# Layernorm tiles transposed in squares by VectorE and through DRAM by DMA, with the w_out products one step later

## The chip, the cores and the metric

The kernel runs on one core of a Trainium2 chip. The metric is the device time of one execution in microseconds (us). The kernel before takes 496.76 us (median of three runs, 496.18 to 496.96). All views below come from one further, profiled execution of 496.89 us, whose traced span is 495.2 us.

## The reference

```python
# attention: batch 2, 8 heads, 768 positions, head_dim 64; keys 0..3 and a window of 128 are seen
scores = where(keep, q @ k.T / 8, -1e9);  a = softmax(scores);  x = a @ v    # -> 1536 tokens x 512
# first MLP: 512 -> 1024 -> 512
h = x @ w_in                      # 1536 x 1024
solu = h * softmax(h)
ln = (solu - mean) / sqrt(var + 1e-6) * g_ln
x2 = ln @ w_out                   # 1536 x 512
# second MLP: 512 -> 2048 -> 512
g = relu(x2 @ w2_in) ** 2
out = g @ w2_out                  # 1536 x 512
```

Everything is float32. Each product of the two MLPs is computed as three products in a rounded format: high by high, high by low and low by high, where "high" is the rounded operand and "low" is what the rounding left.

## The kernel before, in words

The 1536 tokens are 12 tiles of 128. Stage A (until about 224 us of the span) handles attention and the first MLP, in a pipeline written out by hand: `first_step`, `second_step`, then `step(t)` for t = 2 to 9 and `last_step` for t = 10. There is one such function for each engine, and each engine runs its list in order, waiting on semaphores. Stage B (`block_b`) is the second MLP, in three blocks of 512 tokens.

In `step(t)` three tiles are in work. With n = t + 1, TensorE does, in this order: the products of attention weights and values of tile n (`values`, `sink_values`); the transposes of tile t's layernorm (`transpose_ln`, 8 squares of 128 columns, from `u` in SBUF into PSUM); the first two of four pairs of score products of tile t + 2 (`score`); 7 of tile t's 24 w_out products (`project`, of 128x512 each); the other two pairs of scores; the 24 w_in products of tile n (`hidden`); 9 more w_out products; the transposes of tile t + 2's attention weights (`transpose_p`, `transpose_sinks`); the last 8 w_out products.

VectorE (`step`, line 950) does in one step: `square_x2(t - 1)`, which transposes the finished x2 tile in squares of 32x32; `normalize_hidden(t)`, two halves; `split_xT(n)`, the low part of tile n's attention output; three `split_lnT(t, part)`, the low parts of the transposed layernorm, read from PSUM; two `merge`s of scores and `row_max`; `split_q`; two more `merge`s and the second `row_max`; `normalize_p`, `hidden_max`, `split_k` and `gate_and_norm(n)`, which ends in the variance. ScalarE copies scores, rounds (`round_xT`, `round_lnT`), takes the exponentials and copies the transposed weights (`copy_pT`, `copy_sinksT`). GpSimd masks the transposed weights (`halves`) and takes the inverse deviation (`inverse_std`). Tiles 0 and 6 are "alone": they have no earlier keys, so that their score products are smaller and `halves` is left out. The transposed layernorms lie in PSUM banks that are otherwise those of x2 and h.

SyncE issues the loads of q, k and v and `move_x2(t)`: 16 DMAs from SBUF to SBUF, each of 16 KB in runs of 128 bytes, which put the 32x32 squares of x2 in their places in `x2T`, the operand of stage B.

Of the kernel before, what the change touches and what calls it, by code (L numbers as in the profile page):

```python
# [20 lines left out]
P = 128  # L21
# [15 lines left out]
EARLY = 2  # L37
WO_DVE = tuple(k for k in range(F1 // P) if k not in WO_POOL)
# [14 lines left out]
MOVES = 16 * QUADS * QUADS  # L53
# [3 lines left out]
LN_EPS, SM_EPS = 1e-6, 1e-9  # L57

# [11 lines left out]
def chunk_rows(h):  # L70

    return slice(h % 2 * D, (h % 2 + 1) * D), slice(h // 2 * P, (h // 2 + 1) * P)

# [61 lines left out]
def attention_moe_program(nc, qT, kT, v, w_in, w_out, g_ln, w2_in, w2_out, out):  # L135
# [6 lines left out]
    with ctx:  # L142
# [33 lines left out]

        def sbt(name, shape, dt=F32):
            return ctx.enter_context(nc.sbuf_tensor(name, shape, dt))
# [60 lines left out]
        never = sa("never", [P, N_SINK])  # L239
        first = flat(x2T)  # L240
# [50 lines left out]
        lnT_split, xT_split, x2T_moved = sem("lnT_split"), sem("xT_split"), [sem(f"x2T_moved{b}") for b in range(NB)]  # L291
# [4 lines left out]
        lnT_rounded, xT_rounded, x2_squared = sem("lnT_rounded"), sem("xT_rounded"), sem("x2_squared")  # L296
        x2T_rounded, x2T_split = sem("x2T_rounded"), sem("x2T_split")
# [7 lines left out]


# [16 lines left out]
        def _(sp):  # L323
# [19 lines left out]
            def move_x2(t):  # L343

                sp.wait_ge(x2_squared, t + 1)
                squares = squares_of(t).rearrange("p (c r b) -> p c r b", r=QUADS, b=SQ)
                for i in range(QUADS):
                    for r in range(QUADS):
                        sp.dma_start(x2T[r * SQ:(r + 1) * SQ, :, t * P + i * SQ:t * P + (i + 1) * SQ],  # L349
                                     squares[i * SQ:(i + 1) * SQ, :, r, :]).then_inc(x2T_moved[t // TB], 16)  # L350
# [33 lines left out]
            for n in range(3, NT):  # L384
                if n == 5:
                    load_q(n)
                if n >= 5:
                    move_x2(n - 5)
                if n != 5:
                    load_q(n)  # L390
                load_k(n)
                load_v(n - 1)
                if n == 4:
# [4 lines left out]
                if n in range(4, 4 + MC):  # L398
                    c = n - 4
                    sp.dma_start(w2in[:, c, :], w2_in[c * P:(c + 1) * P, :]).then_inc(w2in_loaded, 16)  # L400
            move_x2(NT - 5)
            load_v(NT - 1)
            move_x2(NT - 4)
            move_x2(NT - 3)
# [5 lines left out]
            move_x2(NT - 2)  # L410
            move_x2(NT - 1)
# [165 lines left out]
        def _(act):  # L577
# [54 lines left out]
            def round_lnT(t):  # L632
                done = len(LN_PARTS) * t
                for a, b, place, signals in ln_parts(t):
                    done += signals
                    act.wait_ge(lnT_done, done)
                    nc.scalar.activation(lnT_hi[:, a:b, :], place.rearrange("p (k q) -> p k q", q=P),
                                         ACT.Copy).then_inc(lnT_rounded, signals)
# [17 lines left out]
            def step(t, nxt=True):  # L656
# [7 lines left out]
                if nxt:  # L664
                    copy_earlier(t + 2, 0)
                    copy_earlier(t + 2, 1)
                    bias(t + 2, 0)
                    softmax_exp(t + 2, 0)
                    copy_earlier(t + 2, 2)
                    softmax_exp(t + 2, 1)  # L670
                    copy_earlier(t + 2, 3)
                    softmax_exp(t + 2, 2)
                    softmax_exp(t + 2, 3)
                    finish(t)
# [14 lines left out]
            def first_step():  # L689

                round_xT(1)
                copy_earlier(2, 0)
                copy_earlier(2, 1)
                round_w_out(1, 5)
                copy_earlier(2, 2)
                copy_earlier(2, 3)
                bias(2, 0)
                for h in range(HG):
                    softmax_exp(2, h)
                round_lnT(0)  # L700
                round_w_out(5, len(WO_DVE))
                bias(2, 1)
                for h in range(HG, H):
                    softmax_exp(2, h)
                round_k(3)
                copy_pT(2, 0)
                copy_pT(2, 1)
                hidden_exp(1)
                copy_sinksT(2)

            def second_step():

# [11 lines left out]
                round_lnT(1)  # L724
                finish(1)
# [42 lines left out]
            def round_x2T(blk):  # L768
                cols = slice(blk * BLK, (blk + 1) * BLK)
                act.wait_ge(x2T_moved[blk], TB * MOVES)  # L770
                nc.scalar.activation(x2T_hi[:, :, cols], x2T[:, :, cols], ACT.Copy).then_inc(x2T_rounded, 1)
# [6 lines left out]
            step(NT - 2, nxt=False)  # L778
# [18 lines left out]
            round_lnT(NT - 1)  # L797
# [20 lines left out]
        def _(dve):  # L818
# [99 lines left out]
            def split_lnT(t, part):  # L918
                done = len(LN_PARTS) * t + sum(signals for _, _, _, signals in ln_parts(t)[:part + 1])
                a, b, place, signals = ln_parts(t)[part]  # L920
                dve.wait_ge(lnT_rounded, done)
                nc.vector.tensor_tensor(lnT_lo[:, a:b, :], place.rearrange("p (k q) -> p k q", q=P),  # L922
                                        lnT_hi[:, a:b, :].bitcast(F32), ALU.subtract).then_inc(lnT_split, signals)
# [6 lines left out]
            def square_x2(t):  # L930

                dve.wait_ge(x2_done, t + 1)
                if 0 < t < NT - 1:
                    dve.wait_ge(x2T_moved[(t - 1) // TB], (t - 1) % TB * MOVES + MOVES)
                nc.vector.transpose(squares_of(t), x2_ps[:, :]).then_inc(x2_squared, 1)
# [148 lines left out]
            square_x2(NT - 3)  # L1084
            normalize_hidden(NT - 2)
            split_xT(NT - 1)
            for part in range(len(ln_parts(NT - 2))):
                split_lnT(NT - 2, part)
# [47 lines left out]
        def _(pe):  # L1136
            mm = nc.tensor.matmul

            def score(n, p):
# [6 lines left out]
                if merges(n) and p == 0:  # L1146
                    pe.wait_ge(merged, merges(n))
                if p == 0 and sink_tiles(n):
# [97 lines left out]
            def transpose_ln(t):  # L1246
                if t:
# [9 lines left out]
            def project(t, first, last):  # L1257
                for k, i in x2_products[first:last]:
# [30 lines left out]
            def step(t):  # L1289


                n = t + 1
                values(n, 0)
# [3 lines left out]
                if alone(n):  # L1297
                    score(t + 2, 0)
                    score(t + 2, 1)
                transpose_ln(t)  # L1300
                if not alone(n):
                    score(t + 2, 0)
                    score(t + 2, 1)
# [10 lines left out]
                project(t, 16, 24)  # L1314

            def last_step():
# [4 lines left out]
                sink_values(n)  # L1321
                transpose_ln(n - 1)
                hidden(n, 0, 24)
# [27 lines left out]
            def second_step():  # L1351
# [17 lines left out]
                project(1, 0, 16)  # L1369
# [3 lines left out]
                project(1, 16, 24)  # L1373
# [125 lines left out]
```

## Time and profile before

| what | us |
|---|---|
| median of three runs | 496.76 |
| profiled execution | 496.89 |
| its span | 495.2 |
| TensorE busy | 483.3 (98%) |
| VectorE busy | 284.5 (57%) |
| ScalarE busy | 200.9 (41%) |
| GpSimd busy | 94.3 (19%) |
| stage A, about | 0 to 224 |

Busy time is averaged over the whole span. Stage B is nearly all TensorE, so that VectorE's 57% says little of stage A, where the profile's forty slices show it at eight or nine tenths busy. TensorE's granted clock is at full speed in every slice. The profile's chain that ended last is 82% TensorE and 10% VectorE.

### The profile page before, as it was taken

What the parts mean: (1) busy time and instruction counts of PE and PEld (TensorE: products, weight loads), DVE (VectorE), ACT (ScalarE), POOL (GpSimd) and SP (SyncE); (2) the same over time, 40 slices, a digit from 0 to 9 for tenths busy, and PEclk for the clock granted to TensorE, in tenths of its full rate; (3) what the DMA queues carried; (4) which work ended last, traced back from release to release, by engine and by line L of the source; (5) the groups of instructions that cost most, each with busy time, mean ns of one, the idle gap of its engine ahead of it and who ended that gap; (6) DMA issues with size and microseconds to landing.
All of it is one profiled execution on the core that took longest, in us unless ns stands there. A gap on an engine that the chain in (4) does not pass through costs nothing.

```text
span 495.2 us, 7334 instructions
## 1 busy us (share of the span) xinstructions
PE 483.3 (98%) x2644; PEld 392.8 (79%) x2644; DVE 284.5 (57%) x512; ACT 200.9 (41%) x531; POOL 94.3 (19%) x138
## 2 busy tenths in 40 slices
PE   7989989999999999999999999999999999999997
PEld 5667767888778888878888888888888888888885
DVE  3999888898898888775673554323222332222232
ACT  3667646545655663532334253322112221211221
POOL 2555042120022112267970000000000000000000
PEclk9999999999999999999999999999999999999999
DMA  8921343352222221119100000010000001000002
GB/s 222 309 79 43 134 106 104 124 161 64 59 60 76 53 48 34 17 30 344 29 3 0 1 0 1 34 51 0 0 0 0 0 23 63 0 1 0 0 1 85
DMA packets 39717, 29.21 MB, mean 59 GB/s; under 512 B 29256, under 2 KB 29256, under 8 KB 39176
## 3 DMA queue, kind: packets, MB, share of 16 engines
q1 hardware_dynamic: 39224, 28.30, 19.7%
q10 hardware_dynamic: 464, 0.53, 0.5%
q8 instruction: 18, 0.29, 0.2%
q14 instruction: 11, 0.09, 0.1%
HBM read 22.52 MB, written 3.15 MB: 52 GB/s over the span
## 4 chain that ended last, share of the span: by engine, by line
PE 82%; DVE 10%; SPq 2%; ACT 2%; DMA 1%; issue 1%; POOL 0%; DVEq 0%
PE score_ps L1424 26%; PE h_ps L1438 13%; PE w_ps L1262 10%; PE h_ps L1224 9%; PE wt_ps L1438 7%; PE w_ps L1438 7%; PE o_ps L1194 3%; SPq L349 2%; PE score_ps L1166 2%; PE wt_ps L1174 2%; DVE nmax L850 1%; DVE wo_lo L946 1%; PE wt_ps L1166 1%; PE h_ps L1252 1%; DMA x2T<-kT 1%; DVE prob L915 1%
## 5 line engine op out<-in xcount | busy, mean ns | idle before, releaser
L1424 PE MATMUL score_ps<-x2T_hi,w2in_hi 128*128 (+1 forms) x192 | 74.8, 389 | 0.0
L1424 PE MATMUL score_ps<-x2T_hi,w2in_lo 128*128 (+1 forms) x192 | 74.7, 389 | 0.0
L1424 PE MATMUL score_ps<-x2T_lo,w2in_hi 128*128 (+1 forms) x192 | 74.7, 389 | 0.0
L1099 DVE TENSOR_TENSOR e<-e 128x512 f32<-128x512 f32 x24 | 17.1, 712 | 82.1 <-ACT e L785 82.1
L1099 DVE TENSOR_TENSOR sq<-relu 128x512 f32<-128x512 f32 x24 | 17.7, 738 | 77.9 <-ACT relu L785 77.9
L785 ACT ACTIVATE relu<-score_ps 128x512 f32<-128x512 f32 x24 | 14.4, 598 | 94.2 <-PE score_ps L1424 94.2
L785 ACT ACTIVATE e<-score_ps 128x512 f32<-128x512 f32 x24 | 14.4, 600 | 92.5 <-PE score_ps L1424 92.5
L1424 PEld LDWEIGHTS score_ps<-x2T_hi,w2in_hi 128*128 128x128 f32 x192 | 36.1, 188 | 7.5
L1424 PEld LDWEIGHTS score_ps<-x2T_lo,w2in_hi 128*128 128x128 f32 x192 | 36.0, 188 | 7.5
L1424 PEld LDWEIGHTS score_ps<-x2T_hi,w2in_lo 128*128 128x128 f32 x192 | 36.0, 188 | 7.4
L610 ACT ACTIVATE prob<-sm,nbias 128x132 f32<-128x132 f32 (+1 forms) x96 | 37.9, 396 | 0.5
L1224 PE MATMUL h_ps<-w_hi,xT_hi 128*128 128x512 f32 x88 | 35.6, 405 | 1.3 <-DVE xT_lo L927 1.3
L1262 PE MATMUL w_ps<-wo_hi,lnT_hi 128*128 128x512 f32 x88 | 35.4, 402 | 0.5 <-DVE lnT_lo L922 0.5
L1262 PE MATMUL w_ps<-wo_lo,lnT_hi 128*128 128x512 f32 x88 | 35.2, 400 | 0.0
L1224 PE MATMUL h_ps<-w_hi,xT_lo 128*128 128x512 f32 x88 | 34.4, 391 | 0.0
L1224 PE MATMUL h_ps<-w_lo,xT_hi 128*128 128x512 f32 x88 | 34.4, 391 | 0.0
L1262 PE MATMUL w_ps<-wo_hi,lnT_lo 128*128 128x512 f32 x88 | 34.4, 391 | 0.0
L629 ACT ACTIVATE e<-h_ps,nhmax 128x512 f32<-128x512 f32 x24 | 16.3, 685 | 24.8 <-DVE nhmax L860 24.8
L572 POOL TENSOR_TENSOR w2in_lo<-w2in,w2in_hi 128x512 fp32r<-128x512 f32 x16 | 23.3, 1454 | 1.3
L1224 PEld LDWEIGHTS h_ps<-w_hi,xT_hi 128*128 128x128 f32 x88 | 16.5, 187 | 6.1 <-issue 1.1
L1262 PEld LDWEIGHTS w_ps<-wo_hi,lnT_hi 128*128 128x128 f32 x88 | 16.5, 188 | 5.4 <-DVE lnT_lo L922 1.3
L452 POOL CAST p_sink<-prob 128x64 fp32r<-128x64 f32 x10 | 2.4, 239 | 90.2 <-DVE prob L915 83.3
(182 smaller groups left out, 1105.7 us busy)
## 6 DMA issues: line engine op xcount, KB each, us to landing
w2in<-w_in SPq DMA_DIRECT2D x4, 1024.0 KB, 5.5
w2out<-w_out SPq DMA_DIRECT2D x8, 512.0 KB, 7.5
V<-v SPq DMA_DIRECT2D x12, 256.0 KB, 2.7
x2T<-x SPq DMA_DIRECT2D x176, 16.0 KB, 1.9
k_raw<-kT SPq DMA_DIRECT2D x20, 132.0 KB, 2.8
q_raw<-qT SPq DMA_DIRECT2D x20, 128.0 KB, 2.8
w2in<-w_in SPq DMA_DIRECT2D x4, 512.0 KB, 7.9
w2in<-w_out SPq DMA_DIRECT2D x2, 1024.0 KB, 13.3
```

Of the source, the lines that this page charges most:

```text
L349: sp.dma_start(x2T[r * SQ:(r + 1) * SQ, :, t * P + i * SQ:t * P + (i + 1) * SQ], squares[i * SQ:(i + 1) * SQ, :, r, :]).then_inc(x2T_moved ...
L572: nc.gpsimd.tensor_tensor(w2in_lo[:, :, fs], w2in[:, :, fs], w2in_hi[:, :, fs].bitcast(F32), ALU.subtract).then_inc(w2in_split, 1)
L610: nc.scalar.activation(prob[:, h, seen(n)], sm[:, h, seen(n)], ACT.Exp, bias=nbias[:, h:h + 1], scale=SCALE, accum_out=psum_row[:, h:h + 1 ...
L629: nc.scalar.activation(e[:, cols], h_ps[:, cols], ACT.Exp, bias=nhmax[:, :], scale=1.0, accum_out=hsum[:, half:half + 1]).then_inc(h_exped, 1)
L785: nc.scalar.activation(relu[f % 2], h2_ps[f % 2], ACT.Relu).then_inc(relu_ready, 1)
L1099: nc.vector.tensor_tensor(sq[f % 2], relu[f % 2], relu[f % 2], ALU.mult).then_inc(sq_ready, 1)
L1166: done = mm(score_banks(n, p)[:, j, cols], qs[rows], ks[rows], start=(n < 2 or i == 0), stop=(n < 2 or i == len(products) - 1))
L1194: last = mm(o_ps[rows, cols], V[:, slot, h * D:(h + 1) * D], pT[:, g, j * P:(j + 1) * P], start=(g == 0 and part == 0 and i < 2), stop=(al ...
L1224: done = mm(h_ps[:, cols], xs[:, c, :], ws[:, c, cols], start=(c == 0 and k == 0), stop=(c == MC - 1 and k == 2))
L1262: done = mm(x2_ps[:, :], ls[:, k, :], ws[:, k, :], start=(k == 0 and i == 0), stop=(k == C1 - 1 and i == 2))
L1424: done = mm(h2_ps[f % 2], ws[:, c, fs], xs[:, c, bass.ts(blk, BLK)], start=(c == 0 and i == 0), stop=(c == MC - 1 and i == 2))
L1438: done = mm(y_ps[q], gs[f % 2][:, qs], ws[:, f, :], start=(f == 0 and i == 0), stop=(f == C2 - 1 and i == 2))
```

## The change

For tiles 2 to 9 (`carried`) TensorE no longer transposes the layernorm. Instead VectorE transposes `u` in 32x32 squares into a new SBUF tile `uT` (`square_u`, two instructions of 128x512, after `split_xT`); SyncE stores it to DRAM in two DMAs (`store_u`) and loads it back in four DMAs in runs of 512 bytes, so that the squares fall in their places in `lnT_raw` (`load_lnT`). ScalarE rounds and VectorE splits from `lnT_raw`, in SBUF, one step later. The w_out products of tile t - 1 stand in `step(t)`: 3 before `hidden`, 15 after it, 6 after the transposes. The second step does 12 of tile 1's 24 (`LEAD`), step 2 the other 12, and the last step does tile 9's 24 and tile 10's 24. `score(t + 2, 0)` and `(1)` now open TensorE's step, ahead of `values`. Tiles 0, 1, 10 and 11 are transposed by TensorE as before.

x2 also goes through DRAM: 4 DMAs a tile (`store_x2`) write runs of 128 bytes, and 4 DMAs a block of four tiles load them (`load_x2T`), where there were 16 DMAs a tile.

```diff
-MOVES = 16 * QUADS * QUADS
+MOVES = 16 * QUADS
+def carried(t):
+    return EARLY <= t < NT - 2
@@ SyncE
-            def move_x2(t):
+            def store_x2(t):
                 sp.wait_ge(x2_squared, t + 1)
                 for i in range(QUADS):
-                    for r in range(QUADS):
-                        sp.dma_start(x2T[...], squares[...]).then_inc(x2T_moved[t // TB], 16)
+                    sp.dma_start(x2_dram[:, :, :, cols]..., squares_of(t)[i * SQ:(i + 1) * SQ, :]...
+                                 ).then_inc(x2_stored, 16)
+            def store_u(t):
+                for half in range(2):
+                    sp.wait_ge(u_squared, 2 * (t - EARLY) + half + 1)
+                    sp.dma_start(u_dram[t, half * QUADS:(half + 1) * QUADS, :, :, :]..., uT[:, half, :]
+                                 ).then_inc(u_stored, 16)
+            def load_lnT(t):
+                sp.wait_ge(u_stored, 32 * (t - EARLY + 1))
+                sp.wait_ge(lnT_split, len(LN_PARTS) * t)
+                for r in range(QUADS):
+                    sp.dma_start(lnT_raw[r * SQ:(r + 1) * SQ, :, :], u_dram[t, :, :, r, :]...).then_inc(lnT_loaded, 16)
+            for t in range(EARLY, NT - 2):
+                if t > EARLY:
+                    store_x2(t - 2)
+                load_v(t + 2)
+                store_u(t)
+                if t + 4 < NT:
+                    load_q(t + 4)
+                load_lnT(t)
+                if t + 4 < NT:
+                    load_k(t + 4)
@@ ScalarE, step(t)
+                if t > EARLY:
+                    round_lnT(t - 1, 0)
+                copy_earlier(t + 2, 0)
+                copy_earlier(t + 2, 1)
                 if t + 3 < NT:
                     round_q(t + 3)
                 round_xT(n)
-                round_lnT(t)
...
+                    round_lnT(t - 1, 1)
+                    round_lnT(t - 1, 2)
@@ VectorE
+            def square_u(t):
+                if t > EARLY:
+                    dve.wait_ge(u_stored, 32 * (t - EARLY))
+                for half in range(2):
+                    dve.wait_ge(ln_ready, 2 * t + half + 1)
+                    nc.vector.transpose(uT[:, half, :], u[:, cols].rearrange("p (k r b) -> p r k b", r=QUADS, b=SQ)
+                                        ).then_inc(u_squared, 1)
@@ VectorE, step(t)
-                square_x2(t - 1)
+                if t > EARLY:
+                    square_x2(t - 2)
+                    split_lnT(t - 1, 0)
+                merge(t + 2, 0)
+                merge(t + 2, 1)
                 normalize_hidden(t)
                 split_xT(n)
-                for part in range(len(LN_PARTS)):
-                    split_lnT(t, part)
-                merge(t + 2, 0)
-                merge(t + 2, 1)
+                square_u(t)
+                if t > EARLY:
+                    split_lnT(t - 1, 1)
+                    split_lnT(t - 1, 2)
                 row_max(t + 2, 0)
@@ TensorE, step(t)
+                first = LEAD if t == EARLY else 0
+                score(t + 2, 0)
+                score(t + 2, 1)
                 values(n, 0)
                 values(n, 1)
...
-                transpose_ln(t)
-                project(t, 0, 7)
                 score(t + 2, 2)
                 score(t + 2, 3)
-                pe.wait_ge(lnT_split, len(LN_PARTS) * (t + 1))
+                project(t - 1, first, first + 3)
+                pe.wait_ge(u_ready, 2 * t + 2)
                 hidden(n, 0, 24)
-                project(t, 7, 16)
+                project(t - 1, first + 3, 18)
                 transpose_p(t + 2, 0)
                 transpose_p(t + 2, 1)
...
-                project(t, 16, 24)
+                project(t - 1, 18, 24)
@@ TensorE, last_step
                 sink_values(n)
+                project(n - 2, 0, 24)
                 transpose_ln(n - 1)
@@ TensorE, second_step
-                project(1, 0, 16)
+                project(1, 0, LEAD)
                 transpose_p(3, 0)
                 transpose_p(3, 1)
                 transpose_sinks(3)
-                project(1, 16, 24)
```

## Rows read from the trace of the kernel before

**Rows 1.** Busy time by stretch: stretch, length, then PE, PEld, DVE, ACT, POOL, clock.

```profile
157.27:174.87 17.60, 17.60 (x129) 14.39 (x127) 14.90 (x33) 10.23 (x35) 3.56 (x7) 1.00 0.24 62
```

**Rows 2.** The chain that ended last, step 3: start, length, what, instructions.

```profile
89.06 0.25 PE w_ps L1252 x2
89.30 0.66 PE h_ps L1252 x6
89.96 0.56 PE score_ps L1166 x5
90.52 0.36 PE wt_ps L1166 x6
```

**Rows 3.** VectorE's timeline, step 8: start, length, instruction, idle before and its releaser.

```profile
177.62 0.41 DVE L922 TENSOR_TENSOR lnT_lo<-w_ps,lnT_hi 128x256 fp32r<-128x256 f32 x1
177.95 1.01 DVE L922 TENSOR_TENSOR lnT_lo<-h_ps,lnT_hi 128x256 fp32r<-128x256 f32 x2
178.88 0.44 DVE L838 COPY_PREDICATED sm<-own_seen,score_ps 128x256 f32<-128x256 uint32 x1
...
182.60 0.70 DVE L850 TENSOR_REDUCE nmax<-sm 128x4 f32<-128x528 f32 x1
...
185.67 0.17 DVE L910 TENSOR_SCALAR z_eps<-psum_row 128x4 f32<-128x4 f32 x1 [0.73 <-ACT prob L610]
...
192.31 0.70 DVE L935 STREAM_TRANSPOSE x<-w_ps 128x512 f32<-128x512 f32 x1
```

**Rows 4.** VectorE's timeline in the second step and at the start of step 2.

```profile
53.49 1.00 DVE L894 TENSOR_SCALAR u<-u,moments,rstd 128x512 f32<-128x512 f32 x2
54.41 0.43 DVE L838 COPY_PREDICATED sm<-own_seen,score_ps 128x256 f32<-128x256 uint32 x1
...
55.21 0.70 DVE L850 TENSOR_REDUCE nmax<-sm 128x4 f32<-128x528 f32 x1
55.83 0.68 DVE L904 TENSOR_TENSOR QL<-q_raw,QH 128x512 fp32r<-128x512 f32 x1
56.43 0.71 DVE L935 STREAM_TRANSPOSE x<-w_ps 128x512 f32<-128x512 f32 x1
...
70.03 0.72 DVE L935 STREAM_TRANSPOSE x<-w_ps 128x512 f32<-128x512 f32 x1 [0.50 <-DMA x2T<-x]
70.67 0.96 DVE L894 TENSOR_SCALAR u<-u,moments,rstd 128x512 f32<-128x512 f32 x2
```

**Rows 5.** ScalarE's timeline around the start of step 2.

```profile
66.77 0.29 ACT L622 ACTIVATE p_sinkT<-score_ps 96x128 fp32r<-96x128 f32 x1
...
70.47 0.60 ACT L645 ACTIVATE xT_hi<-o_ps 128x512 fp32r<-128x512 f32 x1 [2.89 <-PE o_ps L1211]
```

**Rows 6.** TensorE's timeline, end of the second step and start of step 2.

```profile
63.85 1.04 PE L1174 MATMUL wt_ps<-ident,prob 128*128 128x128 f32 x8
...
67.28 0.66 PE L1194 MATMUL o_ps<-pT_own,V 128*64 128x128 f32 x8 [0.44 <-POOL pT_own L462]
```

**Rows 7.** VectorE's timeline: second row maximum of step 2, x2 squares of steps 3, 10.

```profile
77.39 0.70 DVE L850 TENSOR_REDUCE nmax<-sm 128x4 f32<-128x528 f32 x1
...
87.44 0.70 DVE L935 STREAM_TRANSPOSE x<-w_ps 128x512 f32<-128x512 f32 x1
...
209.89 0.70 DVE L935 STREAM_TRANSPOSE x<-w_ps 128x512 f32<-128x512 f32 x1
```

**Rows 8.** The chain that ended last, last step.

```profile
213.02 5.69 PE h_ps L1224 x24
218.71 5.44 PE w_ps L1262 x24
```

**Rows 9.** The page's DMA queues: kind, packets, MB, share of 16 engines.

```profile
q1 hardware_dynamic: 39224, 28.30, 19.7%
```

**Rows 10.** The page's DMA issues: count, KB each, median us to landing.

```profile
V<-v SPq DMA_DIRECT2D x12, 256.0 KB, 2.7
```

**Rows 11.** SyncE's queue: start, time of the issues, count.

```profile
158.56 11.16 SPq L349 DMA_DIRECT2D x2T<-x  x16
```

More of the change, by code:

```diff
@@ L72, in chunk_rows, with transposed_before @@
     return slice(h % 2 * D, (h % 2 + 1) * D), slice(h // 2 * P, (h // 2 + 1) * P)
+def transposed_before(t):
+    return sum(not carried(i) for i in range(t))
 def flat(x):
@@ L304, in attention_moe_program, with lnT_chunks, in_squares @@
         block = ctx.enter_context(nc.Block())
+        def lnT_chunks(t, part):
+            a, b, place, _ = ln_parts(t)[part]
+            if not carried(t):
+                return place.rearrange("p (k i b) -> p k i b", i=QUADS, b=SQ)
+            half, k = a // (C1 // 2), a % (C1 // 2)
+            return lnT_raw[:, half * QUADS:(half + 1) * QUADS, k * SQ:(k + b - a) * SQ].rearrange("p i (k b) -> p k i b", b=SQ)
+        def in_squares(x):
+            return x.rearrange("p k (i b) -> p k i b", b=SQ)
         def squares_of(t):
@@ L383, in _, with load_w2_in @@
             load_v_sink(1)
[L384 to L393, printed above, removed]
+            def load_w2_in(c):
+                if c == 0:
                     sp.wait_ge(w_split, MC - 1)
@@ L397, in _ @@
                     sp.wait_ge(wo_split_pool, len(WO_POOL))
[L398 to L404, printed above, removed]
+                sp.dma_start(w2in[:, c, :], w2_in[c * P:(c + 1) * P, :]).then_inc(w2in_loaded, 16)
+            for n in range(3, 5):
+                load_q(n)
+                load_k(n)
+                load_v(n - 1)
+            load_w2_in(0)
+            load_q(5)
+            store_x2(0)
+            load_k(5)
+            for t in range(EARLY, NT - 2):
[8 more added lines that the diff above has]
+                    load_k(t + 4)
+                if t - EARLY + 1 < MC:
+                    load_w2_in(t - EARLY + 1)
+                if t == TB + 2:
+                    load_x2T(0)
+            store_x2(NT - 4)
+            store_x2(NT - 3)
+            load_x2T(1)
             sp.wait_ge(h_done, 2 * NT)
@@ L662, in step @@
                 round_xT(n)
-                round_lnT(t)
[L664 to L674, printed above, removed]
+                if t > EARLY:
+                    round_lnT(t - 1, 1)
+                    round_lnT(t - 1, 2)
+                copy_earlier(t + 2, 2)
+                copy_earlier(t + 2, 3)
+                bias(t + 2, 0)
+                for h in range(HG):
+                    softmax_exp(t + 2, h)
+                finish(t)
             def finish(t):
@@ L699, in first_step @@
                     softmax_exp(2, h)
-                round_lnT(0)
+                for part in range(2):
+                    round_lnT(0, part)
                 round_w_out(5, len(WO_DVE))
@@ L723, in second_step @@
                 softmax_exp(3, 3)
-                round_lnT(1)
+                for part in range(2):
+                    round_lnT(1, part)
                 finish(1)
@@ L775, in round_w2out @@
                 nc.scalar.activation(w2out_hi[:, f, :], w2out[:, f, :], ACT.Copy).then_inc(w2out_rounded, 1)
-            step(NT - 2, nxt=False)
+            round_lnT(NT - 3, 0)
+            round_xT(NT - 1)
+            round_lnT(NT - 3, 1)
+            round_lnT(NT - 3, 2)
+            act.wait_ge(x2_done, NT - 2)
+            for part in range(len(ln_parts(NT - 2))):
+                round_lnT(NT - 2, part)
+            act.wait_ge(lnT_split, len(LN_PARTS) * (NT - 2))
             act.wait_ge(o_done, sink_tiles(NT))
@@ L796, in _ @@
             chain(0, 0)
-            round_lnT(NT - 1)
+            for part in range(len(LN_PARTS)):
+                round_lnT(NT - 1, part)
             act.wait_ge(wo_half_read, 1)
@@ L1246, in transpose_ln @@
             def transpose_ln(t):
-                if t:
+                if t and t != NT - 2:
                     pe.wait_ge(x2_squared, t)
@@ L1257, in project @@
             def project(t, first, last):
+                if t > EARLY - 1 and first == 0:
+                    pe.wait_ge(x2_squared, t)
                 for k, i in x2_products[first:last]:
```

76 lines of the change are left out of this document (50 added, 26 removed).

## The prediction

> **What bounds the kernel now.** I read the busy time by stretch first, then the chain of waits, then each engine's own timeline. In an ordinary step of stage A TensorE is busy for 17.60 of 17.60 us, VectorE for 14.90, at a granted clock of 1.00 [rows 1]. So TensorE sets the step, and the eight layernorm transposes stand on its chain: 0.25 + 0.66 = 0.91 us [rows 2], about 1.0 with the gaps beside them. But VectorE's 14.90 is not 2.70 of free time. Between its work lie waits for ScalarE, such as 0.73 us ahead of z_eps [rows 3], which stay whatever TensorE does, because ScalarE in turn waits for VectorE's row maxima. The question is what VectorE's own loop takes once TensorE needs less.
>
> **TensorE's new step.** It loses 1.0 us and nothing is added: some 16.5 us, if it never waits.
>
> **VectorE's new step.** I lay its list out in the new order, by distances from start to start.
> - From the second row maximum to the x2 squares of the next step nothing changes in order: 182.60 to 192.31, 9.71 us, waits for ScalarE included [rows 3].
> - Squares of x2: 70.03 to 70.67, 0.64 [rows 4].
> - Split of layernorm part 0: 177.62 to 177.95, 0.33 [rows 3]. It now reads SBUF, not PSUM; the split of q, from SBUF, takes 0.60 for twice the width [rows 4], so I change nothing.
> - First two merges: a pair takes 0.80 with the wait of the maximum behind it [rows 4]; no maximum follows here, so twice 0.33, 0.66.
> - Both halves of the normalization: 53.49 to 54.41, 0.92 [rows 4]. The wait for the inverse deviation is covered by the splits and merges now ahead of it.
> - Split of the attention output, as wide as the split of q: 0.60.
> - New: two squares of u. No row shows a transpose that reads SBUF with gaps. The nearest row is the same instruction from PSUM, 0.64, and I take it, twice 1.28. Below, half the normalization of the same tile, 0.46; above, 0.92, twice that, were the gaps to halve the speed. Ends for eight steps of two: 2.9 us less, 4.5 us more.
> - Splits of parts 1 and 2: 177.95 to 178.88, 0.93 [rows 3].
> - First row maximum 0.62, split of q 0.60 [rows 4].
> - Last two merges, with the wait: 0.80. The waits for the score copies that stood here before go, since the scores are made much earlier.
>
> Sum ahead of the second maximum: 0.64 + 0.33 + 0.66 + 0.92 + 0.60 + 1.28 + 0.93 + 0.62 + 0.60 + 0.80 = 7.38. With 9.71 that is 17.09 us, more than TensorE's 16.5. VectorE becomes the bound, and an ordinary step goes from 17.60 to 17.1: 0.5 us gained, not 1.0. TensorE will stand about 0.6 us at the top of each step, for the copy of the transposed sinks, which ScalarE makes behind the exponentials of h, which wait for VectorE.
>
> **Steps 2 to 9.** At the end of the second step TensorE loses 12 products, but gains no time by it: its next scores need the copy that ends at 67.06 [rows 5], so step 2 opens at 67.2 in place of 67.28 [rows 6]. Score pairs take 0.56 + 0.36 = 0.92 [rows 2], and the values and sinks some 3.2 before (67.28 to 70.47, with waits for GpSimd that shrink by the 0.9 us of later start). The rounded attention output is there at about 71.2, its split starts at 71.3. From there 0.60 + 1.28 + 0.62 + 0.60 + 0.80 (step 2 has no squares of x2 and no layernorm splits) gives the second maximum at 75.2, where it was at 77.39, and the x2 squares of step 3 at 75.2 + 9.71 = 84.9, where they were at 87.44 [rows 7]: 2.5 us ahead. Of the seven steps that follow, five are ordinary, 0.5 each; the one that scores the alone tile was already loose on VectorE, I give it 0.2, and the one behind it 0.4. That is 3.1, and the squares of step 10 come at 209.89 - 5.6 = 204.3.
>
> **The last step gives it back.** TensorE has 24 products more there: 5.44 us [rows 8]. Before, it did from 209.89 to 218.71 + 5.44 = 224.15. Now: squares, part 0, normalization, attention split, part 1, that is 0.64 + 0.33 + 0.92 + 0.60 + 0.33 = 2.82, and 0.5 for the wait on the attention output and the way to TensorE, releases its third chunk at 207.6. Then 18 products (0.227 each, 4.09), the transposes (0.91), the w_in products (5.69) and 24 products (5.44): 223.8. Stage A ends 0.3 us earlier. Of some 8 us of transposes taken away, TensorE spends most as waiting: about 5 where products were moved out of the second step and step 2, which VectorE bounds, the rest at 0.6 a step.
>
> **DMA.** SyncE issues 16 pieces of x2 in 11.16 us [rows 11], 0.70 each. In their place come 4 + 2 + 4, 7 us: its queue gets freer. Counted from the x2 squares: u is squared at 4.7, its store issued by 5.5 and landed by 8.2 (2.7 for 256 KB [rows 10]). In the queue q's two loads stand between; they wait for the split of q (6.9) and end at 8.3. The four layernorm loads are issued by 11.1 and landed by 13.8; ScalarE wants them at 17.1. Slack 3.3 us, so I cost the trip at nothing. V, ahead of u in the queue, waits for values made 3 us into the step: no delay. The k loads and w2_in behind it have a step of room. Stage B's x2 blocks are stored a step or more before they are read.
>
> **Small pieces into DRAM.** A tile's x2 is 2048 runs of 128 bytes, 128 for each of 16 DMA engines. All packets of the queue take 19.7% of 16 x 495.2 us over 39224 packets, 0.040 us on average [rows 9]: 5.1 us a tile, with u's store behind them. That alone moves u's landing from 8.2 to 11.3 and the layernorm's to 16.8: just in time. Above, 2048 pieces were issued in 11.16 us without piling up, so at most 0.087 each. The Trainium skill, "DMA: Bandwidth & Descriptors", section "Why small descriptors are slow (HBM only)", says that small descriptors cost extra where DRAM is an end, and not between SBUF and SBUF; its "Specifications" say that below 512 bytes the engine reads, modifies and writes. No row before has such a write; the rule points to the rival below, and its own time would be that rival's.
>
> **Rivals.**
> - *TensorE stays the bound (faster).* If the u squares are nearer 0.46, or VectorE's order absorbs more, the step is 16.5 and seven steps gain 0.6 more: 4.2, so 492.4. For it: VectorE's 14.90 busy plus 1.28 is 16.2. Against it: the sum of 17.09.
> - *The layernorm comes late (slower).* It decides above 0.044 us for a 128-byte write. ScalarE's round and VectorE's split of part 0 stand ahead of the merges in both queues, so every us of delay is one of the step. At 0.052 it is 1 us in seven steps: 503.6. Against it: short pieces are surely below the average of a queue whose other packets carry 2 KB.
> - *The clock falls.* TensorE finishes the second step's products 0.9 us before 63.85, so that after transposes of 1.0 it stands from about 64.0 to 67.2, 3.2 us; its pauses before were under 1 us here, at clock 1.00. At 1.2 GHz the scores and values that follow take some 3 us more, and I give it 3 us: 499.6. The Trainium skill, "TensorE: Matmul & The Clock Gate", section "Why this matters for your kernels", warns of idle gaps between bursts of matmuls. By that rule this pause is what speaks against the change.
> - *VectorE and GpSimd hinder each other more* than in these rows: the shift puts the splits beside GpSimd's masks and, in the last step, its w2_in casts. 0.3 us a step and 1 at the end: 499.6.
>
> **How the numbers follow.** 496.89 - 0.3 = 496.6 for an execution like the profiled one; that one lies 0.13 above the median, so 496.5. Chances: forecast 0.40 (own range 495.0 to 498.5, as 0.1 us of a square moves it by 1.6), TensorE bound 0.32, late layernorm 0.13, clock 0.07, hindrance 0.08. Changes under 0.2% (1.0 us) can't be told from none here. The first splits into 0.08 faster, 0.28 same, 0.04 slower; with 0.31 of the second that makes faster 0.39; same 0.29; slower 0.32. The range goes from 492.4 to 501.0, the upper end of the squares' cost, which leaves out most of the late case and a tail below.
>
> **What the profile after would show.** The forecast: ordinary steps of 17.1 us; VectorE without waits but ScalarE's 0.7; TensorE waiting 0.6 at each step's first score and 3 us before step 2; stage A ending near 223.8; u squares of 0.64 to 0.70. It is wrong if steps are 16.5, if ScalarE waits for DMA before rounding part 0, if the clock shows under 1.00 near 67 us, or if the last step is shorter than 19 us from its x2 squares.

## The result and the profile after

The changed kernel takes 499.54 us (median of five runs, 498.81 to 500.19) against 496.81 us for the kernel before (five runs, 496.18 to 496.96): ratio 1.0057, 95% interval 1.0042 to 1.0072. It is slower by 2.7 us, where I had forecast no difference. Its profiled execution took 500.16 us, span 498.1 us, granted clock 0.997 over the span.

Both profiled executions have GpSimd's inverse deviation of tile 1 at 50.36 us, so their times can be set side by side from there. To compare kernels whose executions start differently, I use one length throughout, "stage A from tile 1": from the start of that instruction to the first product of the second MLP, as the chain that ended last gives it (227.00 after, 224.15 before). It is 173.79 us before and 176.64 after, 2.85 more. Another 0.4 lies outside the span (2.06 us in place of 1.69).

The busy time by stretch (stretch, length, then PE, PEld, DVE, ACT, POOL, each with its instructions, the granted clock, DMA share, GB/s):

```profile
64.00:67.20 3.20, 0.18 (x2) 0.00 (x0) 2.90 (x6) 2.57 (x7) 0.64 (x1) 1.00 0.18 47
67.20:69.00 1.80, 1.72 (x24) 1.62 (x26) 1.69 (x4) 1.05 (x3) 1.70 (x3) 0.90 0.19 67
69.00:72.00 3.00, 3.00 (x27) 2.67 (x23) 2.11 (x7) 0.21 (x1) 1.41 (x3) 0.50 0.00 0
155.22:172.46 17.24, 16.86 (x123) 13.63 (x121) 15.87 (x35) 10.39 (x35) 3.55 (x8) 1.00 0.66 159
```

The last row answers to [rows 1]: the ordinary step shrank from 17.60 to 17.24 us, TensorE is no longer busy all the time, and VectorE is busy for 15.87. The other rows are the surprise. TensorE pauses ahead of step 2. In the pause its granted clock still reads 1.00 (2.4 GHz); in the first 1.8 us of work behind it the mean is 0.90, and then it is 0.50, the 1.2 GHz level, for three microseconds. TensorE's timeline there (start, length, instruction, idle before and its releaser), to be set against [rows 6]:

```profile
63.91 0.27 PE L1302 MATMUL score_ps<-ident,p_sink 128*96 128x128 f32 x1
67.28 0.39 PE L1266 MATMUL score_ps<-KH,QH 64*128 64x260 f32 x2 [3.10 <-ACT p_sinkT L687]
...
68.19 0.74 PE L1294 MATMUL o_ps<-pT_own,V 128*64 128x128 f32 x8
68.72 1.07 PE L1294 MATMUL o_ps<-pT_earlier,V 128*64 128x128 f32 x8
```

A group of eight value products takes 1.07 us in place of 0.66 [rows 6], and VectorE stands for 1.83 us until their rounded result is there (its timeline at step 2 and at the x2 squares of step 3; the rows answer to [rows 7]):

```profile
73.04 0.69 DVE L1017 TENSOR_TENSOR xT_lo<-o_ps,xT_hi 128x512 fp32r<-128x512 f32 x1 [1.83 <-ACT xT_hi L713]
73.65 1.30 DVE L1012 STREAM_TRANSPOSE uT<-u 128x512 f32<-128x512 f32 x2
...
76.86 0.70 DVE L929 TENSOR_REDUCE nmax<-sm 128x4 f32<-128x528 f32 x1
...
79.92 0.17 DVE L989 TENSOR_SCALAR z_eps<-psum_row 128x4 f32<-128x4 f32 x1 [0.69 <-ACT prob L675]
...
86.84 0.72 DVE L1025 STREAM_TRANSPOSE x<-w_ps 128x512 f32<-128x512 f32 x1
```

The two squares of u, the one instruction whose cost no row of before showed, take 1.30 from first start to last end: 73.65 to the maximum at 74.87 is 1.22, 0.61 each.

The other loss is in the last step. VectorE's timeline there, then GpSimd's:

```profile
206.18 0.72 DVE L1025 STREAM_TRANSPOSE x<-w_ps 128x512 f32<-128x512 f32 x1
206.82 0.38 DVE L1001 TENSOR_TENSOR lnT_lo<-lnT_raw,lnT_hi 128x256 fp32r<-128x256 f32 x1
207.12 2.41 DVE L973 TENSOR_SCALAR u<-u,moments,rstd 128x512 f32<-128x512 f32 x2
209.46 0.68 DVE L1017 TENSOR_TENSOR xT_lo<-o_ps,xT_hi 128x512 fp32r<-128x512 f32 x1
210.06 2.11 DVE L1001 TENSOR_TENSOR lnT_lo<-lnT_raw,lnT_hi 128x256 fp32r<-128x256 f32 x2
```

```profile
207.21 0.61 POOL L635 CAST w2in_hi<-w2in 128x512 fp32r<-128x512 f32 x1 [0.35 <-PE o_ps L1311]
207.90 1.34 POOL L637 TENSOR_TENSOR w2in_lo<-w2in,w2in_hi 128x512 fp32r<-128x512 f32 x1
209.20 0.80 POOL L635 CAST w2in_hi<-w2in 128x512 fp32r<-128x512 f32 x1
210.08 1.53 POOL L637 TENSOR_TENSOR w2in_lo<-w2in,w2in_hi 128x512 fp32r<-128x512 f32 x1
```

The same normalization takes 1.00 for its two halves in the last step before and 0.99 in an ordinary step after; here it takes 2.41 beside GpSimd's work on w2_in, and the two splits 2.11 in place of 0.98. The split in between, 0.68, is not touched; it has one operand in PSUM. The Trainium skill, "SBUF — State Buffer", section "SBUF: two separate sides", says that VectorE and GpSimd exclude each other on a shared pair of ports when VectorE runs in a mode of two ports, or reads two operands from SBUF while GpSimd reads SBUF too. These rows agree with it: the two groups that grew have all their operands in SBUF, the one that didn't grow has not. e2 tests it. What it cost is on the chain that ended last, which answers to [rows 8] (start, length, what):

```profile
207.20 2.33 DVE u L973 x2
...
210.52 1.66 PE w_ps L1364 x6
...
212.22 3.02 PE w_ps L1364 x12
215.24 0.87 PE score_ps L1352 x8
216.11 5.46 PE h_ps L1324 x24
221.56 5.44 PE w_ps L1364 x24
227.00 4.09 PE score_ps L1523 x18
```

The page's DMA issues (count, KB each, median us to landing) answer to [rows 10]:

```profile
u_dram<-uT SPq DMA_DIRECT2D x16, 256.0 KB, 3.3
lnT_raw<-u_dram SPq DMA_DIRECT2D x32, 128.0 KB, 2.7
...
x_dram<-x SPq DMA_DIRECT2D x44, 64.0 KB, 2.2
```

A 64 KB piece that is written in runs of 128 bytes lands in 2.2 us, and in steps 3 to 9 neither TensorE, VectorE nor ScalarE waits for a DMA.

### The profile page after: what moved, and what is told of

The parts are those of the page before. It is cut to its first block, busy times and chain, and to the rows that moved or that the text cites. A ratio compares the mean times of both kernels' runs of the same rounds, so it can differ in the third digit from the quotient of the medians.

```text
span 498.1 us, 7178 instructions
## 1 busy us (share of the span) xinstructions
PE 479.3 (96%) x2580; PEld 388.7 (78%) x2580; DVE 293.6 (59%) x528; ACT 201.6 (40%) x531; POOL 93.1 (19%) x138
## 4 chain that ended last, share of the span: by engine, by line
PE 62%; DVE 28%; ACT 6%; issue 3%; POOL 1%; DVEq 0%; POOLq 0%; ACTq 0%
PE score_ps L1523 26%; PE h_ps L1537 13%; PE wt_ps L1537 7%; PE w_ps L1537 7%; ACT prob L675 4%; PE w_ps L1364 3%; DVE nmax L929 3%; DVE bstat L951 2%; DVE u L944 2%; DVE sm L917 2%; DVE lnT_lo L1001 2%; PE h_ps L1324 2%; DVE prob L994 2%; DVE uT L1012 2%; DVE hmax L934 1%
## 5 line engine op out<-in xcount | busy, mean ns | idle before, releaser
L1197 DVE TENSOR_TENSOR e<-e 128x512 f32<-128x512 f32 x24 | 17.1, 712 | 82.1 <-ACT e L863 82.1
L1364 PE MATMUL w_ps<-wo_hi,lnT_hi 128*128 128x512 f32 x88 | 36.4, 414 | 2.0 <-DVE lnT_lo L1001 1.9
L1324 PEld LDWEIGHTS h_ps<-w_hi,xT_hi 128*128 128x128 f32 x88 | 16.5, 188 | 7.9 <-issue 4.7
L1364 PEld LDWEIGHTS w_ps<-wo_hi,lnT_lo 128*128 128x128 f32 x88 | 16.5, 188 | 3.6
```

What stands on the lines that cost most here:

```text
L1197: nc.vector.tensor_tensor(sq[f % 2], relu[f % 2], relu[f % 2], ALU.mult).then_inc(sq_ready, 1)
L1324: done = mm(h_ps[:, cols], xs[:, c, :], ws[:, c, cols], start=(c == 0 and k == 0), stop=(c == MC - 1 and k == 2))
L1364: done = mm(x2_ps[:, :], ls[:, k, :], ws[:, k, :], start=(k == 0 and i == 0), stop=(k == C1 - 1 and i == 2))
```

## The experiments

My theory after the comparison: the step's gain is real, and the loss has two places, the clock behind the pause before step 2 and the meeting of VectorE and GpSimd in the last step. The rival was that the pause and the meeting are only symptoms, and that VectorE's added work delays everything. Later runs ask what bounds the shorter step. All kernels but the two marked "from the kernel before" start from the changed kernel.

| kernel | stage A from tile 1, us | ordinary step, us | median, us | ratio to before, interval |
|---|---|---|---|---|
| before | 173.79 | 17.60 | 496.81 | |
| after | 176.64 | 17.24 | 499.54 | 1.0057 (1.0042 to 1.0072) |
| e1 idle products | 175.13 | 17.25 | 499.79 | 1.0053 (1.0029 to 1.0078) |
| e2 GpSimd later | 174.76 | 17.24 | 498.22 | 1.0019 (1.0005 to 1.0033) |
| e3 both | 173.63 | 17.24 | 497.83 | 1.0020 (1.0004 to 1.0037) |
| e4 one square of u | 171.04 | 16.66 | 494.26 | 0.9942 (0.9918 to 0.9966) |
| e5 from before, q on GpSimd | 173.87 | 17.58 | 496.51 | 0.9990 (0.9977 to 1.0003) |
| e7 e2 + 18 products in the second step | 173.68 | 17.24 | 497.17 | 1.0007 (0.9990 to 1.0023) |
| e8 e7 + q on GpSimd | 171.58 | 17.01 | 496.18 | 0.9984 (0.9960 to 1.0008) |
| e9 from before, x2 by DRAM | 173.42 | 17.57 | 496.34 | 0.9990 (0.9975 to 1.0005) |
| e10 e7 + late splits | 168.65 | 16.46 | 492.33 | 0.9919 (0.9891 to 0.9948) |
| e12 e8 + early maximum | 171.78 | 16.89 | 494.25 | 0.9949 (0.9930 to 0.9968) |
| e11 e7 + all three | 168.18 | 16.47 | 490.86 | 0.9882 (0.9848 to 0.9917) |

The first two columns are of one profiled execution each; each ratio is to the runs of the kernel before on the same chip.

**e1: idle products fill the pause.** Thirteen products of 128x512 whose results nobody reads, behind the second step's transposes.

```diff
                 transpose_sinks(3)
+                for _ in range(13):
+                    mm(o_ps[:, :], wo_hi[:, 0, 0:P], wo_hi[:, 1, :], start=True, stop=True)
```

> The changed kernel, with 13 idle products of 128x512 put into TensorE's pause at the end of the second step; they write o_ps, which the values of the next tile start afresh. Theory (the pause of 3.1 us lets the clock fall to 0.50 for about 4 us, and that makes the attention output of step 2 late): the clock stays at 1.00 from 67 to 73 us, the values of step 2 take about 2.0 us in place of 3.2, the second row maximum of step 2 comes at 75.3 in place of 76.9, and the whole takes 1.6 us less than the changed kernel's 499.5, so 497.9. Rival (the values were late for GpSimd's masks, the clock is a side matter): the maximum stays near 76.9 and the time at 499.5.

The clock stays up, and the value products have their old length:

```profile
67.00:71.00 4.00, 4.00 (x60) 3.57 (x58) 3.63 (x10) 2.00 (x5) 2.34 (x5) 1.00 0.15 38
```

```profile
63.43 3.22 PE L1474 MATMUL o_ps<-wo_hi 128*128 128x512 f32 x13
66.76 0.39 PE L1266 MATMUL score_ps<-KH,QH 64*128 64x260 f32 x2
...
68.16 0.61 PE L1294 MATMUL o_ps<-pT_earlier,V 128*64 128x128 f32 x8
```

Counted from tile 1, the split of the attention output starts 1.66 us sooner (70.90 - 49.88 = 21.02, against 73.04 - 50.36 = 22.68). Of that, 0.5 is lost at once: the split of q behind it takes 1.16 us in place of 0.68, since it now falls beside GpSimd's work on the values of the sinks (VectorE's line, then GpSimd's):

```profile
73.30 1.16 DVE L983 TENSOR_TENSOR QL<-q_raw,QH 128x512 fp32r<-128x512 f32 x1
```

```profile
72.62 1.30 POOL L570 TENSOR_TENSOR v_sink<-v_sink_raw,v_sink 32x512 fp32r<-32x512 f32 x1
```

So the second row maximum of step 2 comes 1.2 us sooner, and that much of stage A is the clock's. Stage A is 1.5 us shorter; the other 0.3 falls in step 3, where hz and hz_eps (told below) are shorter. The total does not show the gain and misses the 497.9 that I expected: of the 499.79 us, 2.67 lie outside the span (median), against 1.99 in the changed kernel, and the median span is 496.9 against 497.6.

**e2: GpSimd's w2_in work later.** It now waits for the last step's splits.

```diff
             pool.wait_ge(w2in_loaded, 16 * MC)
+            pool.wait_ge(lnT_split, len(LN_PARTS) * (NT - 2))
```

> The changed kernel, with GpSimd's split of w2_in beginning only when VectorE has split the layernorm of tile 9. Theory (in the last step the two halves of the normalization take 2.3 us in place of 0.9, and the two splits 2.1 in place of 0.9, because GpSimd's casts and subtractions hold SBUF against them): they take 0.9 each again, stage A ends 1.7 us earlier, 497.8. Rival (the last step hangs on TensorE's 24 more products anyway, and a later w2_in makes stage B late): no gain, 499.5 or more.

Stage A is 1.9 us shorter, and the total 1.3. VectorE's timeline, then the chain:

```profile
205.70 0.72 DVE L1026 STREAM_TRANSPOSE x<-w_ps 128x512 f32<-128x512 f32 x1
206.34 0.38 DVE L1002 TENSOR_TENSOR lnT_lo<-lnT_raw,lnT_hi 128x256 fp32r<-128x256 f32 x1
206.64 0.99 DVE L974 TENSOR_SCALAR u<-u,moments,rstd 128x512 f32<-128x512 f32 x2
207.55 0.68 DVE L1018 TENSOR_TENSOR xT_lo<-o_ps,xT_hi 128x512 fp32r<-128x512 f32 x1
208.15 1.01 DVE L1002 TENSOR_TENSOR lnT_lo<-lnT_raw,lnT_hi 128x256 fp32r<-128x256 f32 x2
```

```profile
208.62 4.37 PE w_ps L1365 x18
```

The squares of x2 to the release of the products are 2.92 us (205.70 to 208.62), where the changed kernel has 4.34 and I had forecast 3.3; and the 18 products run in 4.37 in place of 4.72 with a wait inside. The length of the instructions came back by moving GpSimd alone, so the meeting is the cause. The total, 498.2, is 0.4 above the 497.8 that I expected.

**e3: both edits.**

> Both edits of the two runs before. Theory: the two costs lie at different ends of stage A and add up, 499.5 - 3.3 = 496.2, the forecast's 496.5 within 0.5 us. Rival (they overlap, or something else is late next): above 497.5.

In stage A the two costs add: 176.64 - 173.63 = 3.01 us, e2's 1.88 and 1.13 more for the clock. The median spans say the same: 496.35 in e2, 495.2 here. That leaves the stage 0.16 us shorter than before; the forecast was 0.3. The total still stands 0.20% above before, since 2.53 us lie outside the span, against 1.74 for the kernel before; the median spans, 495.2 and 495.3, are equal. The 497.83 lies above the 496.2 that I expected, and on the rival's side of 497.5. The spans show that nothing in stage A was late next; what the rival did not name is the time outside the span.

**e4: only one of the two squares of u** in steps 2 to 9. It leaves out the upper half of these layernorms; SyncE's store, not shown, sends the lower half twice.

```diff
-                for half in range(2):
-                    dve.wait_ge(ln_ready, 2 * t + half + 1)
-                    nc.vector.transpose(uT[:, half, :], ...).then_inc(u_squared, 1)
+                dve.wait_ge(ln_ready, 2 * t + 2)
+                nc.vector.transpose(uT[:, 0, :], ...).then_inc(u_squared, 2)
```

> The changed kernel with one square transpose of u a step in place of two; it leaves out the upper half of the layernorm of tiles 2 to 9 and stores the lower half twice. Theory (VectorE's own list is the bound of every step): each of the eight steps falls by the 0.61 us of the instruction, ordinary ones from 17.24 to 16.63, and the whole to 494.6. Rival (TensorE, or ScalarE's exponentials, set the step): less than 0.15 us a step, above 498.3.

A step of 16.66 in place of 17.24: 0.58 less for an instruction that stands 0.61 in VectorE's order. So VectorE sets the changed step, and TensorE, busy for 16.60 of 16.60 here, is the next bound right behind it:

```profile
155.00:171.60 16.60, 16.60 (x119) 13.54 (x118) 15.23 (x34) 10.40 (x35) 3.55 (x7) 1.00 0.48 129
```

**e5: the kernel before, with seven splits of q on GpSimd.** It takes 0.60 us a step from VectorE. The other half of the edit, not shown, has GpSimd make the split behind the inverse deviation.

```diff
                 row_max(t + 2, 0)
-                if t + 3 < NT:
-                    split_q(t + 3)
```

> The kernel before, with the split of q of seven steps (0.60 us each) taken from VectorE and given to GpSimd behind the normalization. Theory (in the kernel before TensorE alone sets the step): no gain, steps stay at 17.60 and the whole within 0.5 us of 497.0. Rival (VectorE is a bound there too): 0.3 us or more a step, 495 or less.

Nothing moves: steps of 17.58, TensorE busy for all of them. In the kernel before TensorE alone set the step.

```profile
157.00:174.60 17.60, 17.60 (x127) 14.42 (x126) 14.29 (x32) 10.15 (x36) 4.86 (x9) 1.00 0.24 57
```

**e7: half the pause, without idle work.** On top of e2 (its line is not shown), six more w_out products of tile 1 come into the second step, behind its transposes, and step 2 keeps only its last six (the guard that skips the others there is not shown).

```diff
-LEAD = 12
+LEAD = 18
                 project(1, 0, 12)
                 transpose_p(3, 0)
                 transpose_p(3, 1)
                 transpose_sinks(3)
+                project(1, 12, LEAD)
```

> The changed kernel with the later w2_in of GpSimd, and TensorE's pause filled with useful work: 6 of tile 1's w_out products stand behind the transposes of the second step, the last 6 at the end of step 2. Theory (the pause lets the clock fall, whatever fills it keeps it): clock 1.00 from 67 to 73 us, second row maximum of step 2 as in the kernel with idle products, stage A as long as in the kernel before within 0.5 us, and no product more than before, so 497.1. Rival (a pause of 1.7 us is enough for the clock to fall, or the products delay the scores): 498.2, as without the filling.

TensorE's pause is 1.7 us, its clock stays at 1.00, and the value products behind it take 0.60 to 0.66 us:

```profile
66.26 0.39 PE L1267 MATMUL score_ps<-KH,QH 64*128 64x260 f32 x2 [1.69 <-ACT p_sinkT L688]
```

Here too the split of q takes 1.14 us beside GpSimd. Stage A is as long as in e3, and 1.92 us lie outside the span, not 2.53: 497.17, the same as before. With both losses mended the change is worth nothing, as the forecast had it.

**e8: e7 with the seven splits of q on GpSimd.**

> The kernel of the run before this one, with the split of q of seven steps given to GpSimd. Theory (here VectorE sets the step): each of the seven loses 0.60 us, 17.24 to 16.64, and the whole comes to 497.1 - 4.2 = 492.9, faster than both kernels. Rival (TensorE's own list, 16.5 by the forecast, or GpSimd's hold on SBUF takes it back): 495 or more.

A miss. The step lost 0.23 us, not the 0.60 that left VectorE's list. VectorE's timeline says why:

```profile
158.35 0.70 DVE L936 TENSOR_REDUCE nmax<-sm 128x4 f32<-128x528 f32 x1
159.60 0.17 DVE L996 TENSOR_SCALAR z_eps<-psum_row 128x4 f32<-128x4 f32 x1 [0.55 <-ACT prob L682]
...
161.78 0.17 DVE L996 TENSOR_SCALAR z_eps<-psum_row 128x4 f32<-128x4 f32 x1 [0.45 <-ACT prob L682]
```

A wait of 0.55 for ScalarE's exponentials is new, ahead of the first z_eps; the one ahead of the second fell from 0.69 to 0.45. Together 0.31 us of the 0.60 became waiting; a last 0.06 I did not trace. The exponentials start only at the first row maximum, and nothing ahead of that had become shorter. The rival that GpSimd's hold on SBUF takes the gain back is out: beside GpSimd's split of q (1.29 us) the two squares of u keep their 1.29. VectorE's list is no sum: it is a loop through ScalarE.

**e9: the kernel before, with only x2 through DRAM.** The move of x2 (`store_x2`, `load_x2T`) alone, in place of 16 DMAs a tile.

> The kernel before with x2 alone going through DRAM, as in the change: 4 stores a tile in runs of 128 bytes and 4 loads a block; the layernorms are transposed by TensorE. Theory (x2's way is hidden whichever it takes): no change, within 0.5 us of 497.0, steps of 17.60. Rival (short writes to DRAM hold up q, k and v behind them): slower by 1 us or more, ScalarE waiting for q.

Steps of 17.57 and a ratio of 0.999: that part of the change costs nothing and brings nothing.

**e10: e7 with the layernorm's second and third splits later.** They leave the place ahead of the row maxima, where they take 0.91 us, for the one behind the first `normalize_p`, where VectorE waits for ScalarE's exponentials.

```diff
                 square_u(t)
-                if t > EARLY:
-                    split_lnT(t - 1, 1)
-                    split_lnT(t - 1, 2)
...
                 normalize_p(t + 2, 0)
+                if t > EARLY:
+                    split_lnT(t - 1, 1)
+                    split_lnT(t - 1, 2)
```

> The kernel with the filled pause and the later w2_in, with VectorE's splits of layernorm parts 1 and 2 (0.93 us) moved from ahead of the first row maximum to behind the first half's normalized weights. Theory (a step is the loop of VectorE from row maximum to ScalarE's exponentials and back; what stands ahead of the maxima counts in full, what stands behind them fills the wait of 0.69): the wait ahead of the second z_eps goes, an ordinary step falls by 0.69 from 17.24 to 16.55, seven steps give 4.8, so 492.3. Rival (VectorE's load is the bound as a sum, wherever it stands): no change, 497.1. Second rival (TensorE's w_out products now wait for the splits): 497.5 or more.

As forecast: the step is 16.46 us and the total 492.33. TensorE is busy for all of a step here (16.46 of 16.46 us), so that its own list is the bound again, at the 16.5 of the forecast; what VectorE's loop alone would now take can't be read from this run. The splits stand where the wait was, and the second z_eps waits for nothing:

```profile
157.00 0.17 DVE L990 TENSOR_SCALAR z_eps<-psum_row 128x4 f32<-128x4 f32 x1
...
158.05 1.02 DVE L1002 TENSOR_TENSOR lnT_lo<-lnT_raw,lnT_hi 128x256 fp32r<-128x256 f32 x2
...
159.59 0.16 DVE L990 TENSOR_SCALAR z_eps<-psum_row 128x4 f32<-128x4 f32 x1
```

**e12: e8 with the first row maximum directly behind the first two merges.** If the exponentials' late start is what e8 ran into, this should free it.

```diff
                 merge(t + 2, 1)
+                row_max(t + 2, 0)
                 normalize_hidden(t)
...
-                row_max(t + 2, 0)
                 merge(t + 2, 2)
```

> The kernel with the split of q on GpSimd (steps of 17.01), with the first row maximum moved from behind the layernorm splits to directly behind the first two merges. Theory of the loop: the wait for the exponentials that replaced the split of q (0.55 ahead of the first z_eps) goes, since they now begin 4 us earlier; the split's 0.60 then counts in full and a step falls from 17.01 to 16.64, seven steps 2.6 us, so 493.6. Rival (VectorE's list as a sum): no change, 496.2.

The wait ahead of the first z_eps is gone, but 0.73 us now stand ahead of the second, and the step is 16.89, 0.12 less than in e8, where I had expected 0.37 less (16.64). A miss as well: taking one wait away brought the next one out. The total, 494.25, is 1.9 lower than e8's, while stage A is no shorter in the profiled executions (171.78 against 171.58). Executions of one kernel differ by that much (493.96 to 499.94 in e8), so I take only the step from it.

**e11: e7 with all three edits**, the splits of q on GpSimd, the early maximum and the late splits.

> All edits together: filled pause, later w2_in, split of q on GpSimd, first row maximum behind the merges, layernorm splits behind the normalized weights. Theory: VectorE's loop would need 17.24 - 0.69 - 0.60 = 15.95, so TensorE is the bound again at the 16.5 of the forecast; 497.1 - 7 x 0.74 = 491.9, faster than both kernels by 5 us. Rival (ScalarE's chain or the copy of the sinks sets another bound near 17.0): 495.5 or more.

```profile
155.00:172.00 17.00, 17.00 (x121) 14.12 (x120) 15.65 (x35) 10.95 (x38) 4.98 (x8) 1.00 0.49 133
```

490.86 us (490.62 to 491.53), 1.2% below the kernel before and the best version here. TensorE is busy all the time again, at 16.47 us a step, with VectorE at 15.65 of 17.00. The step is no shorter than e10's, and can't be, since TensorE bounds both: the late splits alone reach that bound, and what the other two edits would give on top is not shown.

## Why the prediction was wrong

**TensorE bounds the kernel before: right.** e5 takes 0.60 us a step from VectorE and the step stays.

**An ordinary step of 17.1, set by VectorE: right.** It measured 17.24, and e4 shows whose bound it is. From the squares of x2 to the second row maximum it takes 7.25 (155.08 to 162.33) where my sum has 7.38; the squares of u were 1.22 for two against 1.28. The stretch from the second row maximum to the next squares of x2 was 9.99, not 9.71 [rows 3]. That row was one of the shortest: in the kernel before the stretch already runs from 9.68 to 10.06 in steps 3 to 9, and I took the row of step 8 for all. VectorE and GpSimd meet in this stretch as well, as VectorE's and then GpSimd's timeline of an ordinary step after show:

```profile
170.08 0.62 DVE L946 SCALAR_TENSOR_TENSOR hz<-hsum 128x1 f32<-128x1 f32 x1
...
171.40 0.58 DVE L956 SCALAR_TENSOR_TENSOR hz_eps<-hz 128x1 f32<-128x1 f32 x1
```

```profile
170.05 0.64 POOL L531 TENSOR_SCALAR_AFFINE_SELECT pT_earlier<-pT_earlier 128x512 f32<-128x512 f32 x1
...
171.34 0.63 POOL L531 TENSOR_SCALAR_AFFINE_SELECT pT_earlier<-pT_earlier 128x512 f32<-128x512 f32 x1
```

The small instruction hz, of one element a partition, ends at 170.70, with the mask that began at 170.05 (ends 170.69); hz_eps ends with the mask of 171.34. In step 8 of the kernel before hz took 0.15 and hz_eps 0.41, at another moment of the masks. Whether the masks hold them is read from these ends and was not tested. TensorE waits 0.19 us at the top of a step for the copy of the sinks (to 152.82) and 0.21 for a merge further on (to 156.51), where I had 0.6 for the copy.

From the squares of step 3 to those of step 10 the trace has 119.3 us (86.84 to 206.18); I had forecast 119.4. That the two agree so well is partly luck. The four ordinary steps among the seven (3, 6, 7 and 8) gained about 0.33 each, not 0.5; step 9, which I had counted as ordinary, has no split of q left to do and gained 0.96 (16.62 us).

**Step 2: the step that failed first.** I had the values take their usual length, the second row maximum at 75.2 and the squares of step 3 at 84.9; they came at 76.86 and 86.84. I had worked out the pause itself rightly (64.0 to 67.2) and then kept what it does to the clock out of the sum, as a rival with a chance of 0.07. The trace has 0.50 behind it, which slows the values that VectorE waits for: the split of the attention output starts at 73.04, 1.7 later than my 71.3, and e1, where the clock stays up, has it 1.66 earlier. From there to the second row maximum I was right within 0.1 (3.82 against 3.90), and the stretch behind it took 9.98 (76.86 to 86.84), 0.27 more than my 9.71: together the 1.9. So the term that failed is the length of the scores and values of step 2, which I took at the full clock. Undoing it gives back only 1.1 to 1.2 us (e1, e3), not 1.66, because the split of q then meets GpSimd; the rival had 3. The rule of the Trainium skill that the prediction weighed there ("TensorE: Matmul & The Clock Gate", section "Why this matters for your kernels") spoke against the change, and this trace agrees with it.

**The last step: the second that failed.** Forecast 19.5 us from the squares of x2 to the second MLP, measured 20.82 (206.18 to 227.00). My terms, 0.92 for the normalization and 0.33 for a split, came from rows where GpSimd left them alone; here the normalization took 2.33 and the two splits 2.11. That is what failed: the lengths were right for their rows, and wrong beside what GpSimd does in this step. In the last step the work on w2_in starts as soon as TensorE's values are done; before, it started 1.7 us behind the squares of x2 (when the normalization was nearly done) and met only splits that read PSUM until 214.99, when the w_in products ran:

```profile
211.58 0.62 POOL L570 CAST w2in_hi<-w2in 128x512 fp32r<-128x512 f32 x1 [0.97 <-PE o_ps L1211]
```

Now it starts 1.0 us behind them (207.21), and meets the normalization and two splits from SBUF. That was a rival too, with a chance of 0.08, at 0.3 us a step and 1 at the end. The 0.3 a step is about what the masks may cost above; the end cost more. e2 has 19.05 without it, 0.5 below my forecast, so that the meeting costs 1.8.

Together: 1.9 late into the last step and 1.3 in it make 3.2 over the forecast's 223.8, which is 227.0. I had treated two unlikely rivals as excluding each other; both happened, at about 1.2 and 1.8 us, and neither alone cost the 3 us that I gave each.

**The gain of the steps given back in the last step: right.** With both losses removed (e3, e7) stage A ends 0.1 to 0.2 us sooner than before, and the total is not faster.

**DMA hidden: right.** The trip through DRAM never made ScalarE wait, at a DMA share of 0.66 in the ordinary step against 0.24 [rows 1], and e9 shows that the writes of 128 bytes don't matter in this kernel. The rival of a late layernorm, to which I gave 0.13, has nothing for it.

**Outside the span: not in the forecast.** I had carried over the 1.69 us of before; the medians are 1.99 after, 1.74 before. It is a tenth of the loss, and its cause is open.

## What to carry to other kernels

When a change takes work away from the engine that sets the pace, work out where that engine then stands idle, and what the pause does to its clock, before counting the gain. When an order is shifted, list what VectorE and GpSimd do at the same moment, above all at the ends of a pipeline, where other work than in its middle runs. And read a bound that passes from engine to engine as a loop: moving 0.91 us of work out of the stretch that the other engine waits for, into the wait that it causes, gave 0.78 us a step (until TensorE was the bound again), while taking 0.60 us out of the same list at another place gave 0.23.

## What the runs showed of the hardware

- A pause of TensorE of 3.10 us was followed by a granted clock of 0.50 (69 to 72 us); in the pause it still read 1.00, and 0.90 on average in the 1.8 us behind it. A pause of 1.69 us in the same place was followed by 1.00. Thirteen products nobody reads, in place of the pause, kept it at 1.00.
- VectorE's 128x512 instructions from SBUF to SBUF took 2.41 us for two beside GpSimd's cast and subtraction on w2_in, 0.99 without; the two splits of 128x256 took 2.11 and 1.01. A split with one operand in PSUM kept its 0.68. The split of q, 128x512 from SBUF, took 1.16 beside GpSimd's work on the sinks (e1), 0.68 without.
- VectorE's instructions hz and hz_eps, of one element a partition, took 0.62 and 0.58 us at one moment of GpSimd's masks, and 0.15 and 0.41 at another; that the masks are the reason was not tested.
- A transpose of a 128x512 tile in 32x32 squares takes VectorE 0.61 us from SBUF, and 0.64 from PSUM, start to start.
- The time outside the span depends on the program: 1.74 us before (median), 1.99 after, 2.67 and 2.53 in the two kernels with idle products, 1.73 in e11. No run here says why, and in e1 and e3 it hid a gain that the spans show.
